# Attention with pooled queries and two feed-forward blocks: output copies on VectorE, blocks of the maximum and the turn rescheduled, seven units for GpSimd

## What is computed

```python
q_pool = q.reshape(B, H, S // 2, 2, D).mean(axis=3)
scores = matmul(q_pool, k.transpose(0, 1, 3, 2)) / sqrt(D)
scores = scores - max(scores, axis=-1, keepdims=True)
attn = exp(scores); attn = attn / (sum(attn, axis=-1, keepdims=True) + 1e-09)
x = matmul(attn, v)              # reordered to 2304 x 512
h = x @ w_in;  x = (h * sigmoid(h)) @ w_out            # 512 -> 2048 -> 512
out = ((x @ w1) * (x @ w2)) @ w3 @ w_out2              # 512 -> 1024 -> 1024 -> 512
```

## Time and profile before

| | us |
|---|---|
| median of 3 runs | 1342.31 (1341.69 to 1344.86) |
| the profiled execution | 1341.67 |
| its span, first to last instruction | 1339.6 |
| attention stage, from the first turn on | 24.6 to 600 |
| TensorE busy over the span | 1292.4 (96%) |
| ScalarE, VectorE, GpSimd busy | 599.6, 592.4, 342.5 |

### The profile page before, as it was taken

The page is one execution under the profiler, slowest core; times in us unless marked ns, Lnnn a source line. Parts: engine busy times, 40 slices in busy tenths (PEclk is TensorE's granted clock), DMA queues, the critical chain, the costliest instruction groups (busy, mean ns, idle before and its releaser), DMA issues.

```text
span 1339.6 us, 26046 instructions
## 1 busy us (share of the span) xinstructions
PE 1292.4 (96%) x10896; PEld 1151.2 (86%) x10896; DVE 592.4 (44%) x886; ACT 599.6 (45%) x1114; POOL 342.5 (26%) x295
## 2 busy tenths in 40 slices
PE   6999999999999999999999999999999999999998
PEld 4999999999999999988888888888998888888888
DVE  6777777777767777733311112111136222222221
ACT  3666666667666666673322222222245121212211
POOL 4556565665656565440000000000000000000000
PEclk9999999999999999999999999999999999999999
DMA  4122222221121211102100000000125000000001
GB/s 136 47 70 71 72 71 72 72 71 49 60 72 54 71 58 50 36 27 64 48 8 1 1 0 1 0 0 0 48 88 180 0 1 32 0 32 0 32 9 40
DMA packets 25300, 58.57 MB, mean 44 GB/s; under 512 B 7136, under 2 KB 7776, under 8 KB 25184
## 3 DMA queue, kind: packets, MB, share of 16 engines
q1 hardware_dynamic: 25184, 56.91, 13.2%
HBM read 52.04 MB, written 4.79 MB: 42 GB/s over the span
## 4 chain that ended last, share of the span: by engine, by line
PE 91%; DVE 3%; ACT 3%; issue 2%; DMA 1%; POOL 0%; ACTq 0%; SPq 0%; DVEq 0%
PE psum L875 18%; PE psum L877 18%; PE psum L876 18%; PE psum L942 17%; PE psum L892 9%; PE psum L921 8%; PE psum L923 2%; DVE mx L682 2%; ACT psum L501 1%; DVE pL L716 1%; ACT tmpB L517 1%; PE psum L903 1%; ACT tmpA L516 1%; ACT qH L522 0%; DMA qraw<-in_qT 0%
## 5 line engine op out<-in xcount | busy, mean ns | idle before, releaser
L682 DVE TENSOR_REDUCE mx<-psum 128x2 f32<-128x768 f32 x240 | 228.6, 957 | 95.8 <-PE psum L892 95.8
L496 ACT ACTIVATE pH<-psum 128x576 fp32r<-128x576 f32 x288 | 188.5, 655 | 179.9 <-PE psum L923 178.9
L942 PE MATMUL psum<-pH,vH 64*128 64x288 f32 x1152 | 196.1, 305 | 25.4 <-ACT tmpB L517 23.2
L421 POOL TENSOR_TENSOR pL<-pF,pH 128x576 fp32r<-128x576 f32 x96 | 137.0, 1427 | 227.3 <-ACT pF L499 227.3
L942 PE MATMUL psum<-pH,vL 64*128 64x288 f32 x1152 | 189.1, 292 | 0.0
L942 PE MATMUL psum<-pL,vH 64*128 64x288 f32 x1152 | 188.7, 291 | 0.0
L812 DVE TENSOR_TENSOR gL<-gF,gH 128x512 fp32r<-128x512 f32 (+1 forms) x80 | 51.4, 642 | 305.2 <-ACT gH L587 305.2
L716 DVE TENSOR_TENSOR pL<-psum,pH 128x576 fp32r<-128x576 f32 x192 | 144.5, 752 | 70.6 <-ACT psum L501 69.1
L584 ACT ACTIVATE gF<-psum 128x512 f32<-128x512 f32 (+1 forms) x80 | 44.4, 555 | 266.8 <-PE psum L877 265.5
L942 PEld LDWEIGHTS psum<-pH,vH 64*128 64x128 f32 x1152 | 127.2, 184 | 41.0 <-issue 30.9
L942 PEld LDWEIGHTS psum<-pH,vL 64*128 64x128 f32 x1152 | 127.4, 185 | 0.0
(11 more groups left out here) (96 smaller groups left out, 2702.5 us busy)
## 6 DMA issues: line engine op xcount, KB each, us to landing
qraw<-in_qT SPq DMA_DIRECT2D x16, 576.0 KB, 4.7
kraw<-in_kT SPq DMA_DIRECT2D x16, 576.0 KB, 3.7
vraw<-in_v SPq DMA_DIRECT2D x16, 576.0 KB, 3.8
rsums<-recips SPq DMA_DIRECT2D x32, 144.0 KB, 3.0
wstage<-in_w_in SPq DMA_DIRECT2D x16, 256.0 KB, 4.7
fstage<-in_w3T SPq DMA_DIRECT2D x8, 512.0 KB, 4.9
w12stage<-in_w SPq DMA_DIRECT2D x8, 512.0 KB, 4.6
outT<-oS SPq DMA_DIRECT2D x4, 1024.0 KB, 4.2
```

Of the source, the lines that this page charges most:

```text
L421: pool.tensor_tensor(pL[r][:], pF[n // 3 % 2][:], pH[r][:].bitcast(F32), ALU.subtract).then_inc(pL_pool, 1)
L496: act.activation(pH[r][:], scores, ACT.Exp, scale=SCALE).then_inc(pH_ready, 1)
L682: dve.tensor_reduce(mx[:, qt, :, kb], bank[:, :, 0:KW], AX.X, ALU.max).then_inc(max_taken, 1)
L942: last = pe.matmul(obank[hd], vals[own(rows_of), c, hd:hd + 2, :].rearrange("p e d -> p (e d)"), probs[own(rows_of), hd, :], start=(c == 0 ...
```

## The change

The copies of the outputs go from ScalarE to VectorE. Items of the maximum run in steps 17, 0, 2 to 9 and 11 to 15. In steps 0, 9 and 17 the block of the maximum comes after both halves of the values, and in step 11 ahead of the scores as in step 2; step 10 has none. The turn, the reduction of the columns and the negation come one step later (17, and 16 on VectorE). `place_even` stands between the two exponentials of unit 17. GpSimd splits units 0, 3, 6, 9, 12, 15 and 16. Some casts on ScalarE and subtractions on GpSimd shift by a step. TensorE's order becomes: step 15: S, V12.1, M, V13.0; step 16: S, V13.1, V14.0; step 17: S, turn, V14.1, V15.0, M; step 0: S, V15.1, V16.0, M; step 1: V16.1, V17.0, S, V17.1; step 2: M, S, V0.0; steps 3 to 8: S, V, M, V; step 9: S, V6.1, V7.0, M; step 10: V7.1, V8.0, S, V8.1; step 11: M, S, V9.0; steps 12 to 14: S, V, M, V.

```diff
--- before.py
+++ after.py
@@ -58,7 +58,8 @@
     ITEM = [(qt, kb) for kb in range(2) for qt in range(2)] + [(0, 2), (1, 2)] + \
            [(qt, kb) for qt in range(2, QT) for kb in range(KB)]
     ITEMS = len(ITEM)
-    ITEM_STEP = {17: 0, 0: 1, **{s: s for s in range(2, ITEMS)}}
+    ITEM_STEP = {17: 0, 0: 1, **{s: s for s in range(2, 10)}, **{s: s - 1 for s in range(11, 16)}}
+    POOL_UNITS = (0, 3, 6, 9, 12, 15, 16)
     RING = 4
     assert NC == 9 and Q <= 1024 and KW <= 512 and ITEMS == QT * KB == 15
 
@@ -249,17 +250,22 @@
 
             return slice(0, min(TILE, TOK - t * TILE))
 
-        LO_POOL = ALL // 3
+        LO_POOL = len(POOL_UNITS) * PAIRS
         LO_DVE = ALL - LO_POOL
 
         def by_pool(n):
 
-            return n % 3 == 0
+            return n % UNITS in POOL_UNITS
+
+        def pool_order(n):
+
+            return n // UNITS * len(POOL_UNITS) + sum(1 for u in POOL_UNITS if u < n % UNITS)
 
         def lo_done(n):
 
-            pools = n // 3 + 1
-            return (pL_pool, pools) if by_pool(n) else (pL_dve, n + 1 - pools)
+            if by_pool(n):
+                return pL_pool, pool_order(n) + 1
+            return pL_dve, n + 1 - pool_order(n)
 
         def item_at(p, s):
 
@@ -418,7 +424,7 @@
                 pool.wait_ge(pH_ready, n + 1)
                 need(pool, pv_done, 2 * (n - RING + 1))
                 r = n % RING
-                pool.tensor_tensor(pL[r][:], pF[n // 3 % 2][:], pH[r][:].bitcast(F32), ALU.subtract
+                pool.tensor_tensor(pL[r][:], pF[pool_order(n) % 2][:], pH[r][:].bitcast(F32), ALU.subtract
                                    ).then_inc(pL_pool, 1)
 
             def w_lo(i):
@@ -457,9 +463,10 @@
                 p_lo(n)
                 if more:
                     k_lo(p + 1, 2)
-                    q_lo(p + 1, 1)
                 if not first:
                     v_lo(p, 1)
+                if more:
+                    q_lo(p + 1, 1)
                 p_lo(n + 3)
                 v_lo(p, 2)
                 if more2:
@@ -476,27 +483,30 @@
                     k_lo(p + 2, 0)
                 if not first:
                     normalize(p - 1, 0, (normalized, 2 * p - 1))
-                p_lo(n + 15)
                 if more2:
                     k_lo(p + 2, 1)
+                p_lo(n + 15)
+                p_lo(n + 16)
                 if more:
                     v_lo(p + 1, 0)
-            normalize(PAIRS - 1, 1, lo_done(ALL - 3))
+            normalize(PAIRS - 1, 1, lo_done(ALL - 2))
             normalize(PAIRS - 1, 0, (normalized, 2 * PAIRS - 1))
 
 
 
         @block.scalar
         def _(act):
-            def exp(n):
+            def exp(n, between=None):
                 r = n % RING
                 act.wait_ge(st_scored, 2 * (n + 1))
                 need(act, pv_done, 2 * (n - RING + 1))
                 scores = stbank[n % 2]
                 act.activation(pH[r][:], scores, ACT.Exp, scale=SCALE).then_inc(pH_ready, 1)
+                if between is not None:
+                    place_even(between)
                 if by_pool(n):
-                    need(act, pL_pool, n // 3 - 1)
-                    act.activation(pF[n // 3 % 2][:], scores, ACT.Exp, scale=SCALE).then_inc(pF_ready, 1)
+                    need(act, pL_pool, pool_order(n) - 1)
+                    act.activation(pF[pool_order(n) % 2][:], scores, ACT.Exp, scale=SCALE).then_inc(pF_ready, 1)
                 else:
                     act.activation(scores, scores, ACT.Exp, scale=SCALE).then_inc(pF_ready, 1)
 
@@ -508,13 +518,6 @@
                 act.copy(mrow[p % 2][:, 0:last].rearrange("p (t e d) -> p t e d", e=2, d=D)[:, :, 0, :],
                          pairbank[0][:, 0, 0:last // 2].rearrange("p (t d) -> p t d", d=D)).then_inc(m_placed_even, 1)
                 act.copy(mrow[p % 2][:, last:Q], pairbank[0][:, 0, last // 2:last // 2 + D]).then_inc(m_placed_even, 1)
-
-            def take_o(p, a):
-
-                act.wait_ge(pv_done, 2 * (UNITS * p + NC * (a + 1)))
-                need(act, normalized, 2 * (p - 1))
-                act.copy(tmpA[p % 2][:, a, :], obank[0]).then_inc(o_taken, 1)
-                act.copy(tmpB[p % 2][:, a, :], obank[1]).then_inc(o_taken, 1)
 
             def q_hi(p, a):
                 act.wait_ge(q_summed, p + 1)
@@ -548,22 +551,16 @@
             for p in range(PAIRS):
                 first, more, more2 = p == 0, p + 1 < PAIRS, p + 2 < PAIRS
                 for u in range(UNITS):
-                    if u == LAG and not first:
-                        take_o(p - 1, 1)
-                    if u == NC + LAG:
-                        take_o(p, 0)
-                    if u == UNITS - 1 and more:
-                        place_even(p + 1)
-                    exp(UNITS * p + u)
+                    exp(UNITS * p + u, p + 1 if u == UNITS - 1 and more else None)
                     if u == 0 and more:
                         k_hi(p + 1, 2)
-                    if u == 1 and more:
+                    if u == 2 and more:
                         q_hi(p + 1, 1)
-                    if u == 9 and more2:
+                    if u == 8 and more2:
                         q_hi(p + 2, 0)
-                    if u == 12 and more2:
+                    if u == 11 and more2:
                         k_hi(p + 2, 0)
-                    if u == 15 and more2:
+                    if u == 14 and more2:
                         k_hi(p + 2, 1)
             def x_hi(t, e, ready, first_done):
 
@@ -576,7 +573,6 @@
             act.wait_ge(vL_ready, KB * PAIRS)
             act.wait_ge(normalized, 2 * (PAIRS - 1))
             x_hi(0, 1, xH_ready, (h_ready, 0))
-            take_o(PAIRS - 1, 1)
 
             def silu(n, r, w):
                 act.wait_ge(h_ready, n + 1)
@@ -718,6 +714,13 @@
             def w_hi(i):
                 dve.wait_ge(wstage_loaded, 16 * (i + 1))
                 dve.tensor_copy(winH[:, i * WSLICE:(i + 1) * WSLICE], wstage[:]).then_inc(winH_ready, 1)
+
+            def take_o(p, a):
+
+                dve.wait_ge(pv_done, 2 * (UNITS * p + NC * (a + 1)))
+                need(dve, normalized, 2 * (p - 1))
+                dve.tensor_copy(tmpA[p % 2][:, a, :], obank[0]).then_inc(o_taken, 1)
+                dve.tensor_copy(tmpB[p % 2][:, a, :], obank[1]).then_inc(o_taken, 1)
 
             def guard_sums(p):
                 dve.wait_ge(sums_packed, 32 * (p + 1))
@@ -748,15 +751,17 @@
                 for u in range(UNITS):
                     n = UNITS * p + u
                     item = item_at(p, u - 1)
-                    if u == 17 and more:
-                        place_odd(p + 1)
                     if item is not None:
                         take_max(*item)
-                    if u == 15 and more:
+                    if u == LAG and not first:
+                        take_o(p - 1, 1)
+                    if u == NC + LAG:
+                        take_o(p, 0)
+                    if u == 16 and more:
                         reduce_max(p + 1)
                     if n > 0 and not by_pool(n - 1):
                         p_lo(n - 1)
-                    if u == 15 and more:
+                    if u == 16 and more:
                         negate_hi(p + 1)
                         negate_lo(p + 1)
                     if u == 1 and not first:
@@ -769,8 +774,9 @@
                         recip(p - 1)
                     if u == 7:
                         w_hi(p)
-                    if u == 16 and more:
+                    if u == 17 and more:
                         v_hi(p + 1, 0)
+                        place_odd(p + 1)
             p_lo(ALL - 1)
 
             def x_lo(t, e, hi_ready, ready):
@@ -780,6 +786,7 @@
                                       ALU.subtract).then_inc(ready, 1)
 
             x_lo(0, 1, xH_ready, xL_ready)
+            take_o(PAIRS - 1, 1)
 
 
             guard_sums(PAIRS - 1)
@@ -957,28 +964,25 @@
                     if u % NC == 1 and n > LAG:
                         values(n - LAG - 1, 1)
                         values(n - LAG, 0)
-                        if item is not None:
-                            score_max(*item)
                         score_t(p, u)
                         values(n - LAG, 1)
                         continue
-                    if u == LAG and item is not None:
+                    if u % NC == LAG and item is not None:
                         score_max(*item)
                     score_t(p, u)
-                    if u == NC + LAG and item is not None:
+                    if u == UNITS - 1 and p + 1 < PAIRS:
+                        turn_max(p + 1)
+                    if u % NC != LAG and n > LAG:
+                        values(n - LAG - 1, 1)
+                    if u % NC not in (0, LAG) and u != UNITS - 1 and item is not None:
                         score_max(*item)
-                    if u == 16 and p + 1 < PAIRS:
-                        turn_max(p + 1)
-                    if u % NC != LAG:
```

(12 more changed lines are left out.)

## The result

| | before | after |
|---|---|---|
| median, us | 1342.7 (1341.69 to 1344.86) | 1312.07 (1311.58 to 1313.08) |
| ratio | 1 | 0.9771, 95% interval 0.9754 to 0.9788 |
| span of the profiled run | 1339.6 | 1310.7 |
| turn to turn, median | 36.25 | 34.23 |
| VectorE, ScalarE, GpSimd busy | 592.4, 599.6, 342.5 | 607.7, 580.6, 365.3 |

What follows compares the result with a forecast made beforehand. TensorE, busy 544.90 of 575.40 us in attention, was taken as the bound. Gains of 7.8 + 4.2 + 10.2 + 1.5 + 7.5 less 3.5 made 27.7 us, so 1314 us, range 1301 to 1327.

Steps and rivals of the forecast that it cites:

- A copy place: Steps 2 and 11: TensorE's loss around the output copies falls to 0.58 us from 1.14 and 0.86.
- What is late next: Behind the copies: pL on VectorE follows the second exponential, so S two units on waits 0.24 us, 0.10 for restart.
- Back-to-back halves: Steps 1 and 10: adjacent value halves of one unit lose 0.35 us each; M between them saves 10.2 us.
- wait of S in step 16: Step 16: scores wait for VectorE's pL, 0.50 us with restart; the later turn removes it, saving 7.5 us.
- new wait at the placing: Step 17: M waits for ScalarE's placing of the maxima, 0.14 us, with restart 0.25, a loss of 3.5 us.
- Ring: Block of the maximum and its reduction turn in 1.94 us; 9 steps lose 0.10 each, one drops out, saving 1.5.
- Cost nothing: GpSimd's seventh unit, 1.43 us more per pair, delays nothing; without cover it would cost 1.43 x 15.
- copies, step 2: First copy place of a pair: loss of 1.14 us becomes 0.58, gaining 0.56 x 14 = 7.8 us.
- copies, step 11: Second copy place of a pair: loss of 0.86 us becomes 0.58, gaining 0.28 x 15 = 4.2 us.
- The ends: Last pair and hand-over to the feed-forward stage: taken at nought, 1 us either way.
- slower case: Rival: VectorE's copies stretch while GpSimd works, 1.10 us each, losing 33 us, 1347; chance 0.06.

Runs made afterwards that it cites:

- Half copies: The changed kernel with VectorE copying only 144 of the 288 columns of each output bank: 1311.49 us, ratio 0.9773.
- third copy: The changed kernel with one more VectorE copy of 288 columns ahead of the two at each place: 1319.53 us, ratio 0.9828.
- moving units 1 and 10: The changed kernel with GpSimd splitting units 1, 4, 7, 10, 13, 15, 16, casts fitted to it: 1305.27 us, ratio 0.9731.
- half maximum: The changed kernel with the maximum for pairs 1 to 15 taken over half of each block of keys: 1298.98 us, ratio 0.9679.
- spread kernel: The changed kernel with blocks of the maximum in steps 4 to 8 and 13 to 15 placed later: 1307.87 us, ratio 0.9744.

## Why the prediction was right, point by point

*Copies.* They take 457 and 447 ns, assumed 0.46, and start 0.37 apart. By the page "VectorE: DVE Perf Modes" of the Trainium skill, in the section on the TRN2 errata, it would be 425: 5 to 7% too little here. Its section on the DRAIN says that the next operation does not start until the pipe is empty, and the prediction took the rows to contradict it; but the same paragraph of the Trainium skill goes on that an operation that is not held starts earlier, and 390.49 against 390.12 + 0.46 shows 0.09 of overlap, as the earlier trace rows did. A copy place was put at 0.58 and costs 0.54 and 0.51. Step 11 lost 0.81 before and not 0.86, so its gain of 0.28 came out with two terms that were each 0.05 to 0.07 too high: that is luck. In the sum the copies stand at 12.0; alone they brought 12.2 in the 14 periods and 14.2 between the medians.

*What is late next.* The prediction named the second exponential, through pL, as what arrives last. Half copies and the third copy confirm it, and moving units 1 and 10 takes the wait away.

*Back-to-back halves.* Put at 0.35 each; undoing the one at step 9 cost 0.42 per pair with its ring step, put at 0.45.

*Turn.* The wait of S in step 16 is gone: put at 0.50, it was 0.53 from starts. The new wait at the placing was oversized: 0.14 with restart 0.25 forecast, while the block starts 0.05 after it is due and loses 0.11 more, 0.16. What was mis-sized is the 0.14 taken from the earlier trace rows for the way from ScalarE to TensorE: here the block starts 0.06 after ScalarE's end (402.63 to 402.69).

*Ring*, the block of the maximum waiting for the reduction of the one before. Put at 0.10 in 9 steps of the kernel before, found at 0.08 to 0.09 in eight of them; the half maximum gives 0.83 per pair in the changed kernel, 0.09 for each of 9 steps. The prediction had one of the nine steps drop out. None did: there were nine before (0, 4 to 9, 13 and 14) and there are nine after (0, 4 to 8, 13 to 15). But the ninth, step 0, lost 0.19 before and loses 0.08 to 0.10 now, so the 0.10 of the sum came out by another way than the one given.

*GpSimd.* "Cost nothing" held as a cost: no wait of TensorE for its pL is listed. But the unit's worth was missed: 6 to 7 us, on VectorE's side. The prediction subtracted 0.67 x 16 of VectorE's work in passing and did not look at who stood behind it in the queue. The sum came out right because the placing was worked out without that pL.

*Sum.* 27.7 us forecast, 28.9 between the spans. Per pair, terms and findings side by side (us; found from the medians of starts over the middle pairs):

| | put at | found |
|---|---|---|
| copies, step 2 | 0.56 | 0.60 |
| copies, step 11 | 0.28 | 0.30 |
| back-to-back halves, steps 1 and 10 | 0.70 | 0.70 |
| wait of S, step 16 | 0.50 | 0.53 |
| ring | 0.10 | 0.10 |
| block behind the placing | -0.25 | -0.16 |
| together | 1.89 | 2.07 |
| turn to turn | | 2.02 |

The found terms are each good to a few hundredths, which is why they add up to 0.05 more than the period. The ends, taken at nought with 1 us either way, gave 0.6.

*Rivals.* VectorE's copies don't stretch beside GpSimd: 444 to 459 ns in all 64, also where GpSimd works beside them (at step 11 it starts to normalise at 390.68, in the middle of the second copy, which takes 0.45). The two lines:

```profile
L722 DVE COPY tmpA<-psum x32: 448/457/459, 47.8 to 570.9; 128x288 f32<-128x288 f32 x32
...
L723 DVE COPY tmpB<-psum x32: 444/447/448, 48.2 to 571.3; 128x288 f32<-128x288 f32 x32
```

That fits the page "SBUF — State Buffer" of the Trainium skill, "Who interferes with whom", which leaves such copies out of the lock. The third copy puts a price of 7 us on 0.37 more, 0.25 per place; to eat up the whole gain, as in the slower case, the copies would have had to cost about 1 us more per place, four times that.

## What to carry to other kernels

When the busiest engine is at 95%, read its waits from start to start against the price of each block: the ring of block and reduction, 12 us, stood in no list of waits, and the others with a part of their size. Read a wait at its own place, not from the mean of all. For every copy that moves to another engine, find the one arrival that comes last behind it before pricing the copy; here shortening the copies further was worth nothing, and moving what queued behind them 6 to 7 us. A unit of work taken off a queue is worth what stands behind it at its place, not its own length.

## What the runs showed of the hardware

The wait from an engine's end to TensorE's start was not one number: 0.14 us behind the copies on either engine, 0.06 behind ScalarE's placing, 0.05 to 0.06 behind pL on VectorE. A block of six matmuls into another bank between two matmuls of an accumulation, as in the spread kernel, took 0.53, as much as a block without a wait elsewhere.
